# A second value product of head a in three passes of halves, with GpSimd making the halves of its values

## The reference

```python
q_rot, k_rot = rotate(q), rotate(k)
scores = scale * q_rot @ k_rot.T
scores = scores - max(scores, axis=-1)
attn = exp(scores)
attn = attn / (sum(attn, axis=-1) + 1e-09)
x = attn @ v                      # then (tokens, 512)
h = x @ w_in
solu = h * softmax(h)
out = (layernorm(solu) * g_ln) @ w_out
```

## Time and profile before

| | |
|---|---|
| median of 3 runs | 483.8 us (483.62 to 483.8) |
| the profiled execution's own time | 483.53 us |
| its span, first to last instruction | 481.8 us |
| PE busy | 473.4 us, 98% |
| DVE busy | 381.4 us, 79% |
| ACT busy | 250.4 us, 52% |
| POOL busy | 236.1 us, 49% |
| granted TensorE clock | 1.00, which is the upper of its two levels, 2.4 GHz |

### The profile page before, as it was taken

The page is one execution under the profiler, slowest core; times in us unless marked ns, Lnnn a source line. Parts: engine busy times, 40 slices in busy tenths (PEclk is TensorE's granted clock), DMA queues, the critical chain, the costliest instruction groups (busy, mean ns, idle before and its releaser), DMA issues.

```text
span 481.8 us, 7983 instructions
## 1 busy us (share of the span) xinstructions
PE 473.4 (98%) x2553; PEld 402.9 (84%) x2553; DVE 381.4 (79%) x591; ACT 250.4 (52%) x397; POOL 236.1 (49%) x307
## 2 busy tenths in 40 slices
PE   7899999999999999999999999999999999999997
PEld 7678888988898889888888878888888888888885
DVE  6867898889889888988896366999897899888731
ACT  4667677777777777777777352032223222322221
POOL 6877666867686768667772021342352121222110
PEclk9999999999999999999999999999999999999999
DMA  8503544645455545445424203233333233322242
GB/s 295 188 12 77 151 147 113 184 131 168 101 156 164 161 116 152 145 123 169 135 71 100 68 6 59 34 83 69 85 87 62 51 51 68 80 57 60 59 81 84
DMA packets 101009, 50.61 MB, mean 105 GB/s; under 512 B 90280, under 2 KB 90280, under 8 KB 99048
## 3 DMA queue, kind: packets, MB, share of 16 engines
q1 hardware_dynamic: 100152, 50.00, 38.7%
q10 hardware_dynamic: 816, 0.10, 0.1%
HBM read 33.33 MB, written 4.79 MB: 79 GB/s over the span
## 4 chain that ended last, share of the span: by engine, by line
PE 95%; DVE 2%; ACT 1%; DMA 1%; issue 0%; SPq 0%; DVEq 0%; ACTq 0%
PE ps L1169 20%; PE ps L1183 20%; PE ps L1155 20%; PE ps L1106 18%; PE ps L1077 8%; PE ps L1135 4%; PE ps L1121 4%; DMA X<-x_in 1%; DVE nm L843 1%; DVE X L780 1%; DVE QK L816 0%; DVE X L785 0%; ACT QK L595 0%; ACT p_main L650 0%; ACT QK L610 0%
## 5 line engine op out<-in xcount | busy, mean ns | idle before, releaser
L843 DVE TENSOR_REDUCE nm<-ps 128x1 fp32r<-128x576 f32 x144 | 108.1, 755 | 31.7 <-PE ps L1077 29.1
L1155 PE MATMUL ps<-p_main,V 128*128 128x288 f32 x404 | 114.8, 406 | 0.0
L1169 PE MATMUL ps<-w_hi,KB 128*128 128x512 f32 x288 | 91.5, 390 | 0.0
L1183 PE MATMUL ps<-w_hi,QK 128*128 128x512 f32 x288 | 91.0, 389 | 0.0
L1106 PE MATMUL ps<-QK 128*128 128x288 f32 x320 | 90.0, 362 | 0.8 <-ACT p_main L650 0.5
L650 ACT ACTIVATE p_main<-ps 128x576 f32<-128x576 f32 x101 | 65.7, 651 | 42.6 <-PE ps L1106 41.2
L1155 PEld LDWEIGHTS ps<-p_main,V 128*128 128x128 f32 x404 | 71.0, 190 | 10.8 <-ACT p_main L650 0.2
L412 POOL TENSOR_TENSOR X<-X,rope 128x1152 f32<-128x1152 f32 x26 | 68.5, 2660 | 10.8 <-POOL v_lo_b L453 8.2
L1106 PEld LDWEIGHTS ps<-QK 128*128 128x128 f32 x320 | 55.6, 189 | 17.9 <-issue 5.7
L1106 PE MATMUL ps<-KB 128*128 128x288 f32 x320 | 67.8, 293 | 0.0
L486 POOL COPY V<-oe 32x256 f32<-32x256 f32 x72 | 29.8, 413 | 74.2 <-DVE QK L894 41.6
(11 more groups left out here) (118 smaller groups left out, 717.8 us busy)
## 6 DMA issues: line engine op xcount, KB each, us to landing
X<-x_in SPq DMA_DIRECT2D x13, 1152.0 KB, 5.1
V<-oe SPq DMA_DIRECT2D x213, 32.0 KB, 1.9
V<-v_in SPq DMA_DIRECT2D x32, 160.0 KB, 2.8
out<-X SPq DMA_DIRECT2D x18, 256.0 KB, 2.3
w_raw<-w_in SPq DMA_DIRECT2D x16, 256.0 KB, 2.9
xT<-x_in SPq DMA_DIRECT2D x2, 1152.0 KB, 10.2
xT<-oe SPq DMA_DIRECT2D x16, 144.0 KB, 2.4
inv<-inv_rows SPq DMA_DIRECT2D x16, 144.0 KB, 3.0
```

The source lines that it names most:

```text
L843: nc.vector.tensor_reduce(nm[g][:, at:at + 1], src[:, :, 0:HALF], AX_XY, ALU.max, negate=True)\
L1155: ins = nc.tensor.matmul(o_ps[a][:, half, 0:HALF], v, p[:, half * HALF:(half + 1) * HALF], start=(k == 0), stop=(k == 9))
L1169: ins = nc.tensor.matmul(h_ps[t % 3][:, half, :], left[a][:, c, :], right[:, col:col + 512], start=(c == 0 and k == 0), stop=(c == KC - 1 ...
L1183: ins = nc.tensor.matmul(y_ps[a], left[a][:, c * P:(c + 1) * P], right[:, col:col + 512], start=(i == 0), stop=(i == DOWNS - 1))
```

## The change

A third tile, k = 1 of head a, joins `HALVED`, in the pairs 2 to 14. Its exponential therefore goes to head b's accumulator in step 1, and ScalarE's copy of the last pair's head b, `take_o(n - 1, 1)`, moves from behind that exponential to ahead of it. VectorE's step 1 gets a `low_p` and loses `low_queries` of head b, which goes to GpSimd, ahead of `rotate`. GpSimd halves v for k = 1 and k = 3 between `rotate` and the high half of the keys; only k = 8 stays at the old place. The buffers and semaphores of the halves of v become three of each kind.

```diff
-HALVED = (3, 8)
+HALVED = (1, 3, 8)
...
         def halved(n, k):
-            return k in HALVED and (1 if k == HALVED[0] else 2) <= n < PAIRS - 1
+            return k in HALVED and (1 if k == HALVED[1] else 2) <= n < PAIRS - 1
```

In GpSimd's list:

```diff
             for n in range(1, PAIRS):
+                if n == 1:
+                    pool.wait_ge(low_q_done[1], 3)
+                elif n + 1 < PAIRS:
+                    pool.wait_ge(low_k_done[1], n + 2)
+                    pool.wait_ge(hi_done[1], high(n + 1, 1))
+                    pool.wait_ge(low_q_done[1], n + 1)
+                    low_queries(n + 1, 1)
+                    pool.wait_ge(low_q_done[1], n + 2)
                 if n + 2 < PAIRS:
-                    pool.wait_ge(low_q_done[1], n + 2)
...
                     rotate(n + 2)
+                for k in HALVED[0:2]:
+                    if halved(n + 1, k):
+                        halve_v(n + 1, k)
                 if n + 2 < PAIRS:
                     pool.wait_ge(rot_done, n + 3)
                     high_keys(n + 2, 0)
...
                     high_keys(n + 2, 1)
-                if halved(n + 1, HALVED[0]):
-                    halve_v(n + 1, 0)
-                    halve_v(n + 1, 1)
+                if halved(n + 1, HALVED[2]):
+                    halve_v(n + 1, HALVED[2])
```

In ScalarE's:

```diff
                 if s != BOTH and halved(n, s + s // BOTH):
                     a = s // BOTH
                     act.wait_ge(o_taken, 2 * n + a)
+                    if s == HALVED[1] and n >= 2:
+                        act.wait_ge(pv_done, PVS * n + HALVED[0] + 1)
...
                 for s in range(STEPS):
+                    if s == 1 and n >= 2:
+                        take_o(n - 1, 1)
                     exp(n, s)
...
-                        if s == 1:
-                            take_o(n - 1, 1)
+                        if s == 1 and n == 1:
+                            take_o(0, 1)
```

In VectorE's:

```diff
-                    if s == 1:
-                        low_queries(n + 1, 1)
+                    if s == 1 and halved(n, HALVED[0]):
+                        low_p(n, HALVED[0])
+                    if n == 1 and s == 1:
+                        low_queries(2, 1)
```

More of the change, by code:

```diff
@@ L89, in attention_then_mlp @@
         p_lo = sb("p_lo", [P, S], F32R)
-        v_hi = [sb(f"v_hi_{h}", [P, P], F32R) for h in "ab"]
-        v_lo = [sb(f"v_lo_{h}", [P, P], F32R) for h in "ab"]
+        v_hi = [sb(f"v_hi{i}", [P, P], F32R) for i in range(len(HALVED))]
+        v_lo = [sb(f"v_lo{i}", [P, P], F32R) for i in range(len(HALVED))]
         oe = [sb(f"oe{c}", [P, 2, S]) for c in range(2)]
@@ L104, in attention_then_mlp @@
         p_lo_done = sem("p_lo_done")
-        v_hi_done = [sem(f"v_hi_{h}_done") for h in "ab"]
-        v_lo_done = [sem(f"v_lo_{h}_done") for h in "ab"]
+        v_hi_done = [sem(f"v_hi{i}_done") for i in range(len(HALVED))]
+        v_lo_done = [sem(f"v_lo{i}_done") for i in range(len(HALVED))]
         second_done = sem("second_done")
@@ L218, in halved, with halves, head @@
         def halved(n, k):
-            return k in HALVED and (1 if k == HALVED[0] else 2) <= n < PAIRS - 1
-        def halves(n, a):
-            return 2 * (n - 1) + a + (1 if n == 1 else 0)
+            return k in HALVED and (1 if k == HALVED[1] else 2) <= n < PAIRS - 1
+        def halves(n, k):
+            i = HALVED.index(k)
+            return 1 if n == 1 else 3 * (n - 2) + i + 2
+        def head(k):
+            return k // 5
         def high(m, a):
@@ L442, in set_tails, with halve_v @@
                 pool.wait_ge(tails_set, 3 * m)
-            def halve_v(m, a):
+            def halve_v(m, k):
+                i, a = HALVED.index(k), head(k)
+                first = 1 if i == 1 else 2
                 pool.wait_ge(v_loaded[m % 2], uses(m) * 32)
[L447 to L455, removed]
+                if m > first:
+                    pool.wait_ge(pv_done, PVS * (m - 1) + k + 1)
+                    pool.wait_ge(v_lo_done[i], m - first)
+                v = V[m % 2][:, a, (k - 5 if a else k + 1), own(a)]
+                nc.gpsimd.tensor_copy(v_hi[i][:, own(a)], v).then_inc(v_hi_done[i], 1)
+                pool.wait_ge(v_hi_done[i], m - first + 1)
+                nc.gpsimd.tensor_tensor(v_lo[i][:, own(a)], v, v_hi[i][:, own(a)].bitcast(F32), ALU.subtract)\
+                  .then_inc(v_lo_done[i], 1)
+                pool.wait_ge(v_lo_done[i], m - first + 1)
             def high_keys(m, a):
@@ L503, in _ @@
                 nc.gpsimd.memset(V[c][:, 1, :, 0:D], 1.0).then_inc(v_const, 1)
[L504 to L507, removed]
+            for i, k in enumerate(HALVED):
+                nc.gpsimd.memset(v_hi[i][:, other(head(k))].bitcast(F32), 1.0).then_inc(v_const, 1)
+                nc.gpsimd.memset(v_lo[i][:, other(head(k))].bitcast(F32), 0.0).then_inc(v_const, 1)
+            pool.wait_ge(v_const, 10)
             nc.gpsimd.memset(expo[:, :], -0.5).then_inc(const_done, 1)
@@ L553, in _ @@
             pool.wait_ge(low_q_done[0], 3)
-            halve_v(1, 0)
+            halve_v(1, HALVED[1])
             for n in range(1, PAIRS):
+                if n == 1:
[6 more added lines that the diff above has]
+                    pool.wait_ge(low_q_done[1], n + 2)
                 if n + 2 < PAIRS:
-                    pool.wait_ge(low_q_done[1], n + 2)
                     if n == 1:
@@ L851, in row_max, with low_p @@
                     nc.vector.transpose(nm_row[g][:, :], nm[g][:, :].bitcast(F32)).then_inc(turned[g], 1)
-            def low_p(n, a):
-                dve.wait_ge(p_hi_done, halves(n, a))
+            def low_p(n, k):
+                a = head(k)
+                dve.wait_ge(p_hi_done, halves(n, k))
                 nc.vector.tensor_tensor(p_lo[:, :].rearrange("p (b c) -> p b c", b=2), o_ps[1 - a][:, :, 0:HALF],
@@ L970, in _ @@
                         low_keys(n + 1, 1)
-                    if s == 1:
-                        low_queries(n + 1, 1)
+                    if s == 1 and halved(n, HALVED[0]):
+                        low_p(n, HALVED[0])
+                    if n == 1 and s == 1:
+                        low_queries(2, 1)
                     if s == 4 and n >= 2:
                         w_low(n - 1)
-                    if s == 3 and halved(n, HALVED[0]):
-                        low_p(n, 0)
+                    if s == 3 and halved(n, HALVED[1]):
+                        low_p(n, HALVED[1])
                     if n == 1 and s == 7:
                         w_low(0)
-                    if s == 7 and halved(n, HALVED[1]):
-                        low_p(n, 1)
+                    if s == 7 and halved(n, HALVED[2]):
+                        low_p(n, HALVED[2])
                     if s == 5 and n + 2 < PAIRS:
@@ L1125, in weigh_tails, with weigh_halves @@
                             ins.then_inc(pv_done, 1)
[L1127 to L1133, removed]
+            def weigh_halves(n, k):
+                i, a = HALVED.index(k), head(k)
+                pe.wait_ge(v_lo_done[i], n if i == 1 else n - 1)
+                pe.wait_ge(p_hi_done, halves(n, k))
+                for part, (v, p) in enumerate(((v_hi[i], p_hi), (v_lo[i], p_hi), (v_hi[i], p_lo))):
+                    if part == 2:
+                        pe.wait_ge(p_lo_done, halves(n, k))
                     for half in range(2):
@@ L1141, in weigh @@
                     if half == 1:
-                        weigh_halves(n, k // 5)
+                        weigh_halves(n, k)
                     return
@@ L1148, in weigh @@
                         pe.wait_ge(v_loaded[c], uses(n) * 32)
-                        pe.wait_ge(v_const, 8)
+                        pe.wait_ge(v_const, 10)
                         pe.wait_ge(max_taken, STEPS)
```

## The result

The changed kernel takes 486.74 us (median of 5 runs, 486.5 to 487.14) against 483.8 (median of 5, 483.62 to 484.01): 1.0061 times the time before, with an interval of [1.0047, 1.0074]. That is 2.9 us slower. The forecast had the mechanism and its direction; it had 1.4 us where the chip shows 2.9.

A forecast was written before the change was run, and what follows sets the result against it. It took GpSimd's round as the new bound, 16.65 us a pair against 16.48 before. Three pairs at -0.09 and ten at +0.17 gave +1.4 us, so 485.2 us as a median; range 482.2 to 488.0.

The forecast's parts named there:

- GpSimd's round: GpSimd's instruction list followed once per pair, waits and collisions included: 16.65 us against TensorE's 16.39, so it bounds; chance 0.62.
- 2.82 + 2.03 + 3.78 + 2.79 + 5.26 = 16.68: GpSimd's stretches in us: rope products' end to keys' high half, to division, to first v copy, to rope products, rope products.
- 3.78: GpSimd's stretch from the division to the first copy of v: 3.85 us before, forecast at 3.78 to 3.85.
- with a few hundredths that overlap, 16.65: Last step of GpSimd's sum: the 16.68 us was lowered to 16.65 a pair for overlap.
- Three pairs at -0.09 and ten at +0.17: Attention pairs: the first one or two and the last halved pair gain, ten lose: -0.27 + 1.7 = +1.4 us.
- TensorE's gain: Product of k = 1: 0.17 us saved by halving, 0.08 lost to a late third pass, net 0.09 a pair, 1.2 in all.
- 0.16 late: Step 1's exponential on ScalarE, behind the moved copy, starts at 137.70 instead of 137.54, assuming a 0.03 gap.
- GpSimd keeps up: Rival: GpSimd's round comes out under TensorE's 16.39, so the time is 482.6 us; chance 0.25.
- Turns without overlap: Rival: each GpSimd-VectorE hand-over costs the other's whole instruction, 0.14 more at each of five; round 17.35, 492 us; chance 0.05.
- the 0.14 of the forecast: GpSimd and VectorE instructions with two SBUF inputs take turns, overlapping by 0.14 us at a hand-over.
- the load of x and the memsets at the start: A later pair's load of x, waiting for the low queries, and two extra memsets on GpSimd were claimed to cost nothing.
- VectorE's `low_p` against its subtraction: VectorE loses a subtraction of 0.71 us and gets a `low_p` of 0.76: no change in its load.

The follow-up runs named there:

- f1: Changed kernel, but GpSimd's low queries of head b cover only 8 of 576 columns from pair 3 on: 483.70 us, 0.9994 of the kernel before.
- h1: Changed kernel, but VectorE's `w_low` covers only 8 of 512 columns for pairs 1 to 12, the rest zero: 483.54 us, 0.9994 of the kernel before.
- g1: Changed kernel, but all three halvings of v stand at the old place, behind the high half of head b's keys: 500.79 us, 1.0346 of the kernel before.
- f4: As f1, with ScalarE's wait for the copied accumulator written ahead of its wait for the scores: 482.58 us, 0.9973 of the kernel before.
- f3: Kernel before, plus only the moves: head b's low queries on GpSimd, v for k = 3 halved behind the rope products; k = 1 stays fp32: 484.77 us, 1.0020.
- h2: Changed kernel, but ScalarE instead of GpSimd makes the two small copies of the queries' tail from pair 3 on: 482.89 us, 0.9982 of the kernel before.
- g3: Changed kernel with only ScalarE's wait for head b's copied result tied to step 1's exponential, as in f4: 486.67 us, 1.0057 of the kernel before.
- f2: Changed kernel, but head b's low queries are back on VectorE in step 1, behind the new `low_p`: 494.96 us, 1.0228 of the kernel before.
- g2: Changed kernel with both the tail copies on ScalarE of h2 and the tied wait of g3: 482.18 us, 0.9962 of the kernel before.

## Why the prediction was right, and where its sizes were off

**The mechanism was right:** GpSimd's round becomes the longer one and TensorE waits for it through VectorE's sum and maximum. Shown by f1 (take the load away and the pair falls to 16.42), by h1 (take VectorE's turn away and it falls as well) and by g1 (make GpSimd's round longer and the pair follows). The changed kernel's profile has what was to be looked for: no idle time ahead of the rope products, the high half of the keys 2.80 behind them (149.42 - 146.62), `w_low` over 1.2, and 0.22 of waiting for VectorE's maximum.

**GpSimd's round, term by term.** Forecast 2.82 + 2.03 + 3.78 + 2.79 + 5.26 = 16.68, measured 2.80 + 2.05 + 3.84 + 2.81 + 5.29 = 16.79. Each term is within 0.06, but four of the five were too small, the largest miss being 3.78, for which the working had a range up to 3.85 and took the lower end. The step that failed is the size of this round: "with a few hundredths that overlap, 16.65". No row stood behind taking 0.03 off; the collisions that the working had counted already held all the overlap there was. Together that is 16.79 - 16.65 = 0.14 a pair, 1.4 us in ten pairs, almost the whole miss. It weighs so much since the loss is the difference of two rounds of about 16.5 us: under 1% of one of them doubled it.

**The pairs.** "Three pairs at -0.09 and ten at +0.17" came out as three at -0.04 and ten at +0.30: 3.0 - 0.1 = 2.8 us in the trace, 2.9 in the medians. The count of ten was right. But the forecast had two gaining pairs at the start and the last one, and what came was three at the start: the last was 0.32 longer.

**TensorE's gain** was 0.09 forecast, and is 0.06 where GpSimd lets it show (f1). The term that was too small is the exponential "0.16 late": it is 0.25 late, since it follows the copy by 0.12 instead of 0.03 as long as its wait for the copy stands behind others in the list (f4). With the wait tied, the gain is 0.11 to 0.13 (pairs of 16.37 and 16.35 against 16.48), a little over the forecast. In the changed kernel this counted for 3 pairs only.

**The rivals.** "GpSimd keeps up" is f1's kernel, not the changed one; its 482.6 would have been 483.7. "Turns without overlap" put the round at 17.35 and is refuted by 16.79. The hand-over is read in the fences above: `w_low` ends at 145.66 + 1.50 = 147.16, and GpSimd's copy behind it, which takes 0.24 alone, ends at 146.57 + 0.69 = 147.26; so it began its work at 147.02, 0.14 before the other's end. After the sum it is 0.15: that ends at 149.18, and the subtraction of 0.32 at 149.35. That is the 0.14 of the forecast. The Trainium skill (SBUF — State Buffer, "Who interferes with whom") calls the shared port pair an exclusive lock, held for the whole instruction. The lock is here, in h1 most clearly; at the scale of 0.1 us the measured overlap at both ends decides, and that was the difference between 16.8 and 17.35.

**What had no cost as forecast:** the load of x and the memsets at the start (all that lies outside the pairs is 0.1 us), and VectorE's `low_p` against its subtraction (14.20 busy before, 14.25 after).

## What to carry to other kernels

An engine's idle time in a pair is not room for work: in f3 GpSimd idles 1.56 in each round and still sets the pace. Follow its list once round, with every wait that another engine ends and every collision on what they share, and compare that round with the one that sets the pace; the difference of two such rounds is uncertain by as much as the sum of all its terms' small errors. GpSimd and VectorE's instructions with two operands in SBUF are one resource here: work moved between the two only pays by the difference of their durations, and can cost, while two copies of 0.24 moved to ScalarE, which is outside of it, turned a loss of 2.9 us into a gain of 0.9 (h2). A gain that another bound hides, as the tied wait of f4, is worth trying again once that bound is gone.

## What the runs showed of the hardware that wasn't expected

- An exponential of ScalarE that waits for ScalarE's own copy starts 0.12 after the copy's end when this wait stands behind others in the list (f1, the changed kernel), and 0.03 after it when it stands first (f4, g3). That the first wait is tied to the instruction and a later one isn't is the reading that fits; no trace shows the waits themselves.
- VectorE's instruction of 128 x 8 took 0.48 at the end of GpSimd's rope products (h1). A subtraction of 8 columns alone isn't in these traces on VectorE; on GpSimd it took 0.20.
- Once in seven of the kernels the gap between `take_o` and the exponential of step 1 is longer: about 0.40 instead of 0.12 in the changed kernel, f1, f2, g1 and h1, and 0.20 instead of 0.03 in f4 and g3. It is in pair 12 in all seven, which have the same instructions in ScalarE's list, and makes that pair longer by about 0.3 (0.16 in f4). In the changed kernel the next pair gives it back (the 0.59 and 0.01 above), as GpSimd's round goes on at 16.79. In h2 and g2, where ScalarE has two more instructions a pair, no such gap is seen. So it goes with the place in ScalarE's list and not with the time; what it is, no run tells.
